# New order of SyncE's loads of the value means, GpSimd's key copies spread over three half tiles, and a bank of its own for the last tile's gates, in an attention and two-MoE kernel on one core

## The reference

```python
# q, k, v: (4 batches, 8 heads, 768 positions, 64), float32; block 32, window 16
k_sum = k.reshape(B, H, 24, 32, 64).max(axis=3)       # key maximum of each block
v_sum = v.reshape(B, H, 24, 32, 64).mean(axis=3)      # value mean of each block
scores_l = q @ k.T / 8, kept only where |pos_q - pos_k| < 16
scores_s = q @ k_sum.T / 8 + log(32)
a = softmax(concat(scores_l, scores_s))
attn = a @ concat(v, v_sum)                            # -> x: 3072 tokens x 512
# first MoE: a skip score, the expert of the largest logit, x + gate * relu(x @ w1[e]) @ w2[e]
# second MoE: each of 8 experts takes 384 tokens by the order of all logits, relu(x @ w1[e]) @ w2[e]
```

## Time and profile before

| | |
|---|---|
| median of 3 executions | 815.14 us (813.34, 815.14, 815.98) |
| profiled execution | 818.46 us, of which 816.4 us from the first to the last instruction |
| granted TensorE clock, mean | 0.941 of full speed |
| busy: PE / PEld | 731.3 us (90%) / 508.6 us (62%) |
| busy: DVE / ACT / POOL | 361.0 (44%) / 220.0 (27%) / 189.0 us (23%) |
| chain of work that ended last | PE 80%, DVE 8%, issue 3%, DMA 3%, SP's queue 2%, POOL 1% |
| DMA | 119.89 MB, of 130483 packets 95874 are under 512 B |

### The profile page before, as it was taken

The page is one execution under the profiler, slowest core; times in us unless marked ns, Lnnn a source line. Parts: engine busy times, 40 slices in busy tenths (PEclk is TensorE's granted clock), DMA queues, the critical chain, the costliest instruction groups (busy, mean ns, idle before and its releaser), DMA issues.

```text
span 816.4 us, 13908 instructions
## 1 busy us (share of the span) xinstructions
PE 731.3 (90%) x4566; PEld 508.6 (62%) x4566; DVE 361.0 (44%) x1477; ACT 220.0 (27%) x685; POOL 189.0 (23%) x253
## 2 busy tenths in 40 slices
PE   4788998999499999999329999999999999999995
PEld 3688898899378767766215555554555555455552
DVE  3467585888611112112784736546373663600000
ACT  3667676787001111111001111111111111121210
POOL 7465444653111111111110110202011020211001
PEclk8899999999689999999557999999999999999999
DMA  9898968478791517900043612407052160752001
GB/s 222 199 185 198 208 175 193 121 180 274 250 393 66 189 61 272 375 21 8 2 143 104 228 57 87 185 13 258 26 193 91 46 226 14 258 182 103 26 0 39
DMA packets 130483, 119.89 MB, mean 147 GB/s; under 512 B 95874, under 2 KB 95874, under 8 KB 130240
## 3 DMA queue, kind: packets, MB, share of 16 engines
q1 hardware_dynamic: 115312, 87.71, 35.1%
q10 hardware_dynamic: 9360, 15.47, 6.2%
q0 software_dynamic: 5760, 16.03, 5.6%
HBM read 105.95 MB, written 16.50 MB: 150 GB/s over the span
## 4 chain that ended last, share of the span: by engine, by line
PE 80%; DVE 8%; issue 3%; DMA 3%; SPq 2%; POOL 1%; ACTq 1%; ACT 0%; POOLq 0%; DVEq 0%
PE bank L1178 21%; PE bank L1193 20%; PE bank L1059 9%; PE bank L1076 9%; PE bank L933 4%; PE bank L912 4%; PE bank L1111 2%; PE bank L955 2%; PE bank L922 2%; DMA weights<-in_v 1%; DVE scratch L1409 1%; PE bank L1140 1%; PE bank L1039 1%; PE bank L899 1%; DVE shared L1420 1%
## 5 line engine op out<-in xcount | busy, mean ns | idle before, releaser
L1178 PE MATMUL bank<-scratch,weights 128*128 128x384 f32 x512 | 177.6, 499 | 0.1
L1193 PE MATMUL bank<-weights,scratch 128*128 128x512 f32 x384 | 175.2, 600 | 0.0
L1178 PEld LDWEIGHTS bank<-scratch,weights 128*128 128x128 f32 x512 | 94.5, 192 | 63.5 <-issue 10.1
L1193 PEld LDWEIGHTS bank<-weights,scratch 128*128 128x128 f32 x384 | 69.6, 190 | 70.7 <-issue 68.4
L1267 ACT ACTIVATE scratch<-shared,neg_max 128x120 f32<-128x120 f32 x192 | 73.4, 383 | 30.3 <-DVE neg_max L1420 17.7
L1371 ACT ACTIVATE scratch<-bank 128x384 f32<-128x384 f32 x64 | 31.4, 491 | 153.5 <-PE bank L1178 153.5
L689 POOL TENSOR_TENSOR scratch<-scratch,row_inv 128x480 f32<-128x480 f32 x48 | 47.3, 986 | 83.5 <-DVE row_inv L1430 83.3
L1059 PEld LDWEIGHTS bank<-mix,weights 128*128 128x128 f32 x512 | 60.7, 196 | 5.2 <-issue 5.2
L1059 PE MATMUL bank<-mix,weights 128*128 128x128 f32 x512 | 61.5, 279 | 1.4 <-DVE mix L1649 1.4
L933 PE MATMUL bank<-shared,mix 120*128 120x128 f32 x384 | 53.2, 283 | 9.5 <-issue 6.5
L850 POOL DMA_INDIRECT out<-scratch,idx x24 | 24.4, 1015 | 148.8 <-ACT scratch L1377 147.0
(11 more groups left out here) (245 smaller groups left out, 943.8 us busy)
## 6 DMA issues: line engine op xcount, KB each, us to landing
weights<-in_moe_w SPq DMA_DIRECT2D x20, 2048.0 KB, 7.7
scratch<-in_moe_w SPq DMA_DIRECT2D x8, 2048.0 KB, 10.3
weights<-in_moe_w ACTq DMA_DIRECT2D x16, 512.0 KB, 5.4
mix<-in_v SPq DMA_DIRECT2D x40, 192.0 KB
rows<-row SPq DMA_DIRECT2D x24, 264.5 KB, 3.2
scratch<-in_q SPq DMA_DIRECT2D x24, 256.0 KB, 4.4
weights<-in_k SPq DMA_DIRECT2D x21, 256.0 KB, 5.0
weights<-in_v ACTq DMA_DIRECT2D x24, 192.0 KB, 3.6
```

The source lines that it names most:

```text
L1178: last = mm(hb2[f % 2][:, 0:CAP], w1_sb[odd][:, c, f * P:(f + 1) * P], xT2[odd][:, c, :], start=(c == 0), stop=(c == C - 1), skip_group_ch ...
L1193: last = mm(yb2[c % 2][:, :], hT2[odd][:, f, c * P:(c + 1) * P], w2_sb[odd][:, f, :], start=(f == 0), stop=(f == FC - 1), skip_group_check ...
```

## The change

Three edits, independent of one another in code.

1. SP: at w = 4 `keep_means(b + 1)` goes ahead of the tile's store and query load; the wait for `v_sum_out` and the loads of the means move from w = 5 (ahead of the key tiles) to w = 4 (behind the key tiles), and cover half tiles 0 and 1 only; the means of n = 2 to 5 are loaded behind their windows (before: those of n = 4 and 5).
2. POOL: `edges` is split in `left_edges` and `right_edges`. For batch 1 nothing moves. For batches 2 and 3 the left edges stay behind `scale` of n = 7, the right edges go behind that of n = 8, and `maxima` behind that of n = 9 instead of n = 8.
3. The last tile's gates go to bank 1 and no longer wait for `logits_made`; DVE's copies of them read bank 1.

```diff
--- before.py
+++ after.py
@@ -548,26 +548,26 @@
 
             for t in range(NT):
                 b, w = t // TB, t % TB
+                if w == 4 and b + 1 < B:
+                    keep_means(b + 1)
                 if t >= 2:
                     store_tile(t - 2)
                 if t + 4 < NT:
                     sp.wait_ge(s.q_turned, t + 2)
                     load_queries(t + 4)
-                if w == 4 and b + 1 < B:
-                    keep_means(b + 1)
-                if b + 1 < B and w == 5:
-                    sp.wait_ge(s.v_sum_out, 64 * (b + 2))
-                    for g in range(NH * (b + 1), NH * (b + 1) + 4):
-                        load_means(g)
                 if b + 2 < B:
                     for j in ((), (), (0,), (1,), (2, 3), (4, 5))[w] if b == 0 else (w,):
                         sp.wait_ge(s.k_turned, TB * b + j + 1)
                         load_k(b + 2, j)
+                if b + 1 < B and w == 4:
+                    sp.wait_ge(s.v_sum_out, 64 * (b + 2))
+                    for g in range(NH * (b + 1), NH * (b + 1) + 2):
+                        load_means(g)
                 for g in (2 * t + VR, 2 * t + 1 + VR):
                     if g < HT:
                         sp.wait_ge(s.attended, g - VR + 1)
                         load_window(g)
-                        if g >= NH and 4 <= g % NH < 6:
+                        if g >= NH and 2 <= g % NH < 6:
                             load_means(g)
             store_tile(NT - 2)
             store_tile(NT - 1)
@@ -667,12 +667,16 @@
                 nc.gpsimd.tensor_scalar(v_mean[b % 2][0:HB, groups, :], v_blocks[b % 2][0:HB, groups, 0:D], 1.0 / BLOCK, None,
                                         ALU.mult).then_inc(s.v_mean_made, 1)
 
-            def edges(b):
+            def left_edges(b):
 
                 pool.wait_ge(s.kT_vector, k_vector(TB * (b + 1)))
                 pool.wait_ge(s.kT_scalar, k_scalar(TB * (b + 1)))
                 x = kwin[b % 2]
                 nc.gpsimd.tensor_copy(x[:, :, 1:NH, 0:WINDOW], x[:, :, 0:NH - 1, QH:QH + WINDOW])
+
+            def right_edges(b):
+
+                x = kwin[b % 2]
                 nc.gpsimd.tensor_copy(x[:, :, 0:NH - 1, WK - WINDOW:WK], x[:, :, 1:NH, WINDOW:2 * WINDOW])
 
             def maxima(b):
@@ -689,7 +693,8 @@
                 nc.gpsimd.tensor_tensor(out=x, in0=x, in1=inv, op=ALU.mult).then_inc(s.p_scaled, 1)
 
             FOLDS = 5
-            edges(0)
+            left_edges(0)
+            right_edges(0)
             maxima(0)
             pool.wait_ge(s.blocks_in2, 16)
             for step in range(FOLDS):
@@ -755,9 +760,14 @@
                         for step in range(2, FOLDS):
                             fold(nx, step, slice(0, 2))
                         average(nx, slice(0, 2))
-                    elif n == (8 if b == 0 else 7):
-                        edges(nx)
-                    elif n == (9 if b == 0 else 8):
+                    elif n == 8 and b == 0:
+                        left_edges(nx)
+                        right_edges(nx)
+                    elif n == 7:
+                        left_edges(nx)
+                    elif n == 8:
+                        right_edges(nx)
+                    elif n == 9:
                         maxima(nx)
                 if h == HT - 14:
                     constants_a()
@@ -879,6 +889,7 @@
             qx = bank[6]
             kx = bank[7]
             lg = bank[7][:, 0:NL]
+            lg_last = bank[1][:, 0:NL]
 
             def turn_k(kk, to):
 
@@ -949,10 +960,10 @@
 
                 pe.wait_ge(s.xT_a, 2 * t + 2)
                 pe.wait_ge(s.xT_b, 2 * t + 2)
-                if t:
+                if 0 < t < NT - 1:
                     pe.wait_ge(s.logits_made, t)
                 for c in range(C):
-                    last = mm(lg, xT_att[t % 2][:, c, :], gate_weights[:, c, :], start=(c == 0), stop=(c == C - 1),
+                    last = mm(lg_last if t == NT - 1 else lg, xT_att[t % 2][:, c, :], gate_weights[:, c, :], start=(c == 0), stop=(c == C - 1),
                               skip_group_check=True)
                 last.then_inc(s.gates_done, 1)
 
@@ -1449,7 +1460,7 @@
 
             def copy_logits(t):
                 dve.wait_ge(s.gates_done, t + 1)
-                lg = bank[7][:, 0:NL]
+                lg = bank[1 if t == NT - 1 else 7][:, 0:NL]
                 v_.tensor_copy(logits[:, t, :], lg[:, E:NL]).then_inc(s.logits_kept, 1)
                 if t < NT - 1:
                     copy_gates(t)
```

## The result

The changed kernel takes 807.64 us (median of 5 executions, 805.35 to 809.54), before 813.34 us (5, 812.36 to 815.98): ratio 0.9928, 95% interval 0.9906 to 0.9950. That is 5.7 us less by the medians and 5.9 us (4.1 to 7.6) by the ratio. A second set gave 807.03 against 814.09 us, ratio 0.9926 (0.9898 to 0.9953): 7.1 us less by the medians and 6.0 us (3.8 to 8.3) by the ratio. The forecast was 9.7 us less, outside both intervals: the sign is right and the time lies within the range, but the gain is about two thirds of what was forecast. The time itself was missed by 2.1 us only (805.5 forecast), because the median of before, which the forecast was subtracted from, stood at 815.14 us after three executions and at 813.34 us after five. That was luck. Its profiled execution took 805.35 us with a span of 803.3 us, 13.1 us less than before's span.

The account below looks back on a forecast made before the run. PE was taken to bound the kernel, losing time in gaps and half clock. Gaps and clock 8.81, edit 2 0.42 and edit 3 0.50 sum to 9.7 us, taken from 815.14 for 805.5 us, range 801.8 to 811.5.

Parts of the forecast that it names:

- What bounds: PE, busy 90% of the span, idles 4.11 and 2.37 us ahead of the first attend of batches 1 and 2, awaiting means.
- Times of edit 1: On SP, first means issued at 69.0 instead of 75.27 us in batch 1, at 116.8 instead of 122.77 in batch 2.
- The write's landing: Last write of the means lands 2.78 us after issue, so SP does not wait; upper bound 7.52 us.
- What the gaps cost: PE at the first attend of batches 1 and 2: gaps 4.11 and 2.37 us, half clock 1.11 and 1.22, together 8.81.
- The sum for the profiled execution: Whole kernel: 8.81 us for gaps and clock, 0.42 for edit 2, 0.50 for edit 3; 818.46 becomes 808.8 us.
- The clock behind the gaps: PE behind both gaps: each DMA wait brings half clock, 1.11 and 1.22 us; if by chance, only the gaps count.
- Edit 2: PE's gap at n = 9 falls from 0.56 to 0.35 us in two batches, 0.42 us saved, range 0 to 0.42.
- the slowing of the next L1428 by the maxima: DVE at n = 10: L1428 starts within 0.1 us of the maxima's end; if caught, edit 2 would come to 0.
- Edit 3: Last tile's gates no longer start 0.50 us late behind DVE's L1462; 0.50 us gained, at least 0.
- The backlog was handed on: Rival: DMA backlog of 4.3 us makes a new 1.5 us gap in two batches, 810.7 us; 0.18 with late-write case.
- given back later: Rival: low clock at the expert lists' or second MoE's start lasts longer, up to 3.3 us lost, 809 us; chance 0.08.
- Half of edit 1 costed at nothing: SP's early keep_means at w = 4 was given no gain of its own, only earlier loads of the means.

Follow-up runs that it names:

- means_late: Kernel of before with the four loads of the means at w = 5 put behind the key tiles; 818.67 us against 814.24, ratio 1.0057.
- load_first: Changed kernel with keep_means put back behind the store and the queries of w = 4; 806.59 us against 814.24, ratio 0.9916.
- before_again: Kernel of before, no edit, profiled a second time; that execution took 811.33 us.
- rest_only: Kernel of before with edits 2 and 3 only, SP's list as before; 813.13 us, ratio 0.9988.
- write_first: Kernel of before with only keep_means moved to the head of w = 4, means loaded at w = 5 as before; 810.47 us, ratio 0.9967.
- after_again: Changed kernel, no further edit, profiled once more; that execution took 809.33 us against 805.35 in its first profile.
- before_fourth: Kernel of before, no edit, profiled a fourth time; that execution took 815.72 us.
- before_third: Kernel of before, no edit, profiled a third time; that execution took 810.89 us.

## Why the prediction was right, and where its size was wrong

- *What bounds.* Right: PE's gaps ahead of the first `attend` of batches 1 and 2, ended by the means. It had been argued by leaving out the other inputs; means_late and load_first show it.
- *Times of edit 1.* Right. Counted from the mark, the write was forecast 2.2 us ahead of it in batch 1's case and came 2.2 us ahead (60.55 against 62.73); the first means were forecast at 3.8 us behind it and came at 4.1 us, in batch 2's case 3.3 forecast and 2.9 found. The write's landing, taken at 2.78 us, held SP nowhere in batches 1 and 2; in the last batch it held SP 0.7 us. Where SP did wait for a write, there and in load_first, the write took about 3.6 and 3.4 us from the start of its last part (estimates as above), so 2.78 us was low.
- *What the gaps cost.* This is the step that failed, in size: the "8.81 us" were read from one execution and taken for the kernel's. Four profiles of before have stretches 9.15, 3.96, 4.38 and 5.60 us longer than the changed kernel's, 5.8 on average where 9.23 (8.81 and the 0.42 of edit 2) was forecast, and the timed gain is 5.9 and 6.0 us by the two ratios. I had even seen that the profiled execution lay 3.3 us above the median and subtracted the same 9.7 us from the median: an execution that is slower than the others owes its surplus to something, and where a gap ended by DMA is what the change removes, the surplus may be in it. Here it was: its stretch is 3.6 to 5.2 us longer than those of the three others, whose times are 2.7 to 7.6 us below its own.
- *The sum for the profiled execution.* 9.23 us against 9.15 looks like a hit, but it is one by luck, as errors in it cancel. From the start of `turn_p` to that of `attend` at the first half tile the old profile takes 4.71 and 2.97 us (82.79 - 78.08, 129.41 - 126.44) and the new one 0.44 both times, so the gaps cost 6.80 us and not the 6.48 of the brackets. The half clock costs 1.54 and 1.64 us and not 1.11 and 1.22, by before_again's pairs of 3.16 and 3.17 us. Against that, the changed kernel's pairs take 3.80 and 3.79 us, 0.64 and 0.62 more than these, with the new wait for DVE's copy of a key tile, which was not foreseen. So 6.80 + 3.18 - 1.26 + 0.42 = 9.14 us.
- *The clock behind the gaps.* It is not paid each time: in the other three profiles of before it was paid in batch 1 twice and in batch 2 never. The sum without it, which the prediction set beside the other, would be 7.4 us, nearer to what was measured, though the gaps in it are still the long ones of that one execution.
- *Edit 2.* Right: gap 0.56 to 0.35 us, L1428 0.38 to 0.16 us, first score unhindered, and the slowing of the next L1428 by the maxima, for which the prediction weighed the rule of the Trainium skill (GPSIMD Engine Reference, "Key points"), did not come: it took 0.16 us at 106.70, when the maxima's copy was at its end (105.59 and 1.15 us).
- *Edit 3.* Its wait of 0.50 us is gone, as forecast. That the chain behind it moves up by as much is not shown: from the start of the last gates but one to the first expert's matmuls the four profiles of before take 21.03, 21.17, 21.30 and 21.63 us, and those with edit 3 20.82, 21.35 and (rest_only) 21.29.
- *The rivals.* The backlog was handed on, as far as the DMA share shows (1.16 in the place of the gap, 1.20 in batch 2), but no new wait for DMA came of it. What came instead is small and was not foreseen: 0.49 us for DVE's copy of a key tile ahead of `turn_k`, 0.48 in batch 2; before, this copy lay inside the gap. Nothing was given back later: from the third mark to the end the changed kernel takes 654.6 and 656.3 us, before 656.1, 656.1, 655.5 and 656.3.
- *Half of edit 1 costed at nothing.* The prediction took the early write only as what makes early loads possible. write_first shows that by itself it is worth 2.7 us (0.33%, interval 0.09 to 0.58%), as far as its rows go through the earlier issue of what follows it; load_first, that it adds nothing measurable beside the loads' move.

## What to carry to other kernels

A gap that a DMA ends is not a number but a spread: look at two or three executions before it goes into a sum, and if the profiled one is slower than the median, compare how long the stretch around the gap takes in each, by a mark that they all have. To price half clock, take the same steps at full clock, and look whether the pair that you compare with holds a wait of its own; here 0.27 us passed over made the price 0.43 us too low each time. When a load comes late behind full DMA engines, look at when the work ahead of it was issued as well as at the load itself: four writes of 12 KB took the issuing engine 3.2 us or more here, and so belong where that engine waits anyway.

## What was not expected of the hardware

- The same load of the means, behind full DMA engines, took 7.52, 6.6, 6.0 and 6.8 us from issue to use in the four profiles of before, 5.3 us in write_first, and 3.6 us when issued 4.3 us later in the same stretch.
- The clock did not follow the length of the gap alone. Behind or within gaps of 4.56, 4.11, 3.24, 2.68, 2.62, 2.53, 2.52 and 2.37 us at the first `attend` of a batch it fell to 0.50; behind one of 3.25 us, and behind all there of 1.55 us and less, it stayed at 1.00. Ahead of tile 4's queries it fell behind waits of 1.66, 1.75 and 1.99 us (before, after_again, before_fourth) and not behind one of 1.46 us (means_late) or the shorter ones.
- Four writes of 12 KB cost SP 3.23 (changed kernel, 146.50) to 4.44 us of issue (before_third, 111.12), more than two key tiles and a window together in before_third (1.98 and 0.93 us), which carry 704 KB. The issue of key tiles is not always so short: in means_late two took 4.13 us.
